# Outer products of keys and values: one head at a time in column halves, behind the chunk's value products, into the even heads' score bank

## The chip, the core and the metric

The kernel runs on one core of a Trainium2 chip. The metric is the device time of one execution in microseconds (us). TensorE, written PE in the profile, multiplies matrices: it loads a stationary operand (LDWEIGHTS, the rows PEld), streams a moving operand past it (MATMUL), and writes PSUM, eight banks of 2 KB in each of 128 partitions. VectorE (DVE) and ScalarE (ACT) read PSUM and SBUF, GpSimd (POOL) works on SBUF, and SyncE (SP) issues the DMAs. Engines wait for one another on semaphores.

## The reference, cut to what matters

Inputs are q, k, v and alpha of shape (4 batches, 8 heads, 768 steps, 48), and the weights of two feed-forward layers. All is float32.

```
for t in range(S):
    state = alpha[:, :, t, :, None] * state + np.einsum('bhd,bhe->bhde', k[:, :, t], v[:, :, t])
    y[:, :, t] = np.einsum('bhd,bhde->bhe', q[:, :, t], state)
x = y laid out as (3072 tokens, 384)
x = (sigmoid(x @ w_gate) * (x @ w_val)) @ w_out          # 384 -> 1536 -> 384
out = maximum(maximum(x @ w1, x @ w2), x @ w3) @ w_out2  # 384 -> 768 -> 384
```

## The kernel before

**Attention by chunks.** The recurrence runs in chunks of 128 steps (24 chunks; six make a batch). For a chunk, VectorE clamps alpha and scans it to running products (`decay`), and takes reciprocals (`rdec`); GpSimd multiplies q by `decay` and k by `rdec`. TensorE then does five things. `scores` multiplies k by q in each of the eight heads, even heads into bank `ps_sc`, odd heads into `ps_sc_odd`. `transposes` turns k from feature-major to token-major in PSUM, and ScalarE copies it to `khs`. `outer` multiplies `khs` by v, which is the sum over the chunk of outer products k v. `attend` adds two products into `ps_y`: q times the incoming `state` (L775), and v times the masked scores `probs` (L779). VectorE's `masked` makes `probs`, and its `new_state` adds the outer products to the state and multiplies by the decay at the chunk's end. ScalarE copies `ps_y` to the input of the next layer (`y_copy`).

**Two heads side by side.** Heads sit in pairs: one in partitions 0 to 47, one in partitions 64 to 111, with a gap of 16. `outer` takes a pair in one matmul: 112 columns of `khs` as stationary operand, 96 columns of v as moving operand. Half of what it computes (the key of one head by the value of the other) is not read. The products of L779 go one head at a time: 48 columns of v are stationary, and the two heads of a pair write partitions 0 to 47 and 64 to 111 of one bank, so each uses one half of the array's columns. The same split is in `HALVES`.

**The layers.** The first layer works on tiles of 384 tokens (three chunks), eight tiles. A tile has 12 steps f = 0 to 11. A step is 9 matmuls for the gate (`ps_gate`), 9 for the value (`ps_val`), and 9 for the output of the step before (`out1`, L815, into `ps_out`); each product is made of a high and a low part of the operands, hence w_hi, w_lo, x_hi, x_lo. Into tiles 0 to 6 the attention of the next tile's three chunks is woven: behind the gate product of steps 2, 5 and 8 come `scores` and `transposes`, behind the value product of the same steps comes `outer`, and behind the value product of steps 3, 6 and 9 comes `attend`. That is 21 chunks; the first three are done ahead of tile 0. Tile 0 is written out, tiles 1 to 6 are three turns of a loop over two tiles, tile 7 is written out. Then comes the second layer, six tiles of 512 tokens.

**What sets the order.** Each engine's program is written by hand in order, and the engines meet on counted semaphores: `y_done` (attend), `u_done` (outer), `state_done` (two for each new_state), `y_evac` (y_copy), `khs_done` (the copy of k). In the loop `transposes`, `outer` and `attend` all use the bank `ps_y`, so `attend` waits for the new_state of its own chunk. SyncE loads chunk C into the buffer of chunk C-2 as soon as the `attend` of chunk C-2 is done.

Of the kernel before, what the change touches and what calls it, by code (L numbers as in the profile page):

```python
# [32 lines left out]
B, H, S, D = 4, 8, 768, 48  # L33
# [25 lines left out]
def build(nc, att_in, alpha_flat, vT, w1, w2, consts, y, out):  # L59
    with ExitStack() as ctx:  # L60
# [76 lines left out]
        def buf(Cs):  # L137

            return 2 if Cs == 2 else Cs % 2
# [10 lines left out]
        def v_cols(b, lo, n):  # L150
            return buf_cols(b, ATT + lo, n)

        def u_bank(Cs, i):

            if isinstance(i, int) and Cs < CPT:
                return ps_out[:, 1, :]
            return ps_y.rearrange("p a t -> p (a t)")

        def arrived(eng, sems, Cs, i):

            if Cs == 2:
                eng.wait_ge(sems[2], 16)
            elif Cs < 2:
                eng.wait_ge(sems[Cs], 16)
            else:
                eng.wait_ge(sems[Cs % 2], (Cs // 2 + Cs % 2 + 3 * i) * 16)
# [38 lines left out]
        def _(sp):  # L205
            def load_chunk(Cs, i):
                b, a = buf(Cs), PAIRS * CH
                if isinstance(i, int) and Cs in (3, 4):
                    sp.wait_ge(y_done, 5 - Cs)
                elif not (isinstance(i, int) and Cs < 3):  # L210
                    sp.wait_ge(y_done, Cs + 6 * i - 1)
                sp.dma_start(buf_cols(b, 0, a), att_in[Cs + 6 * i][:, 0:a]).then_inc(alpha_loaded[b], 16)
                sp.dma_start(buf_cols(b, a, INC - a), att_in[Cs + 6 * i][:, a:INC]).then_inc(att_loaded[b], 16)

# [104 lines left out]
            for j in range(NF2):  # L319
                if j >= 2:  # L320
                    sp.wait_ge(w2_hi_done, j - 1)
                    sp.wait_ge(w2_lo_done, j - 1)
                else:
                    sp.wait_ge(y_done, CHUNKS)
                sp.dma_start(inbuf[:, (j % 2) * INC:(j % 2) * INC + W2C], w2[j]).then_inc(stage2_in[j % 2], 16)
            with sp.Fori(0, TILES2 - 1) as T:
                sp.wait_ge(o_evac, T * SUB + SUB)
# [209 lines left out]
        def _(dve):  # L537
# [38 lines left out]
            def new_state(Cs, i):  # L576

                C, cur, new = Cs + 6 * i, Cs % 2, (Cs + 1) % 2
                dve.wait_ge(u_done, C + 1)
                dve.wait_ge(end_done, C + 1)  # L580
                for n, r in enumerate(HALVES):
                    u = u_bank(Cs, i)[r, 0:PAIRS * 2 * D].rearrange("p (a e) -> p a e", a=PAIRS)[:, :, n * D:(n + 1) * D]
                    end = d_end[r, cur, :].rearrange("p (a e) -> p a e", e=1).broadcast_to([D, PAIRS, D])
                    e = slice(r.start, r.stop)
                    if Cs % (2 * CPT) == 0:
                        nc.vector.tensor_tensor(state[r, new, :, e], u, end, ALU.mult).then_inc(state_done, 1)
                        continue
                    dve.wait_ge(state_done, 2 * C)
                    nc.vector.tensor_tensor(stmp[r, :, :], u, state[r, cur, :, e], ALU.add).then_inc(stmp_done, 1)
                    later = Cs - Cs // (2 * CPT) - 1 + 5 * i  # L590
                    dve.wait_ge(stmp_done, 2 * later + n + 1)
                    nc.vector.tensor_tensor(state[r, new, :, e], stmp[r, :, :], end, ALU.mult).then_inc(state_done, 1)
# [11 lines left out]
            def layer1(Ts, i, att_next):  # L604
                T = Ts + 2 * i
                C0 = CPT * (Ts + 1)
                for f in range(NF1):
                    g = T * NF1 + f
                    c = f // 3
                    att = (C0 + c, i) if att_next and c < CPT else None  # L610
                    if att and f % 3 == 0:
                        scans(*att)
                        recips(*att, (0,))
                    elif att and f % 3 == 1:
                        recips(*att, (3,))
                    elif att:
                        masked(*att, 0)
                        masked(*att, 1)
                    dve.wait_ge(val_done, g + 1)
                    dve.wait_ge(sig_done, g + 1)  # L620
                    dve.wait_ge(h_lo_done, g)
                    nc.vector.tensor_tensor(h_sb[:, :], act_sb[:, :], ps_val[:, 0:TOK], ALU.mult).then_inc(h_done, 1)  # L622
                    if f == NF1 - 1:
                        for k in range(KT):
                            x_rest(k, (T + 1) * KT + k, *((x_raw[:, k, :],) if att_next else (mid_tile2(0, k), TOK2)))
                    h_rest(f, h_hi_done, h_lo_done, g, h_sb[:, :], TOK)
                    if att and f % 3 == 0:
                        recips(*att, (1, 2))
                    elif att and f % 3 == 2:
                        new_state(*att)  # L630

            def general():
                with dve.Fori(0, B * PAIRS) as n:
# [89 lines left out]
        def _(pe):  # L723
            mm = nc.tensor.matmul

            def transposes(Cs, i):
                C, par = Cs + 6 * i, Cs % 2
                pe.wait_ge(kh_done, 2 * C + 2)
                if not (isinstance(i, int) and Cs == 0):
                    pe.wait_ge(state_done, 2 * C)  # L730
                if not (isinstance(i, int) and Cs < CPT):
                    pe.wait_ge(y_evac, C)
                for p in range(PAIRS):
                    ins = nc.tensor.transpose(u_bank(Cs, i)[:, p * PR:(p + 1) * PR], att(buf(Cs), K)[:, p, :],  # L734
                                              ident[0:PR, 0:PR])
                ins.then_inc(tr_done, 1)

            def scores(Cs, i):

                C = Cs + 6 * i  # L740
                pe.wait_ge(qh_done, C + 1)
                if not (isinstance(i, int) and Cs == 0):
                    pe.wait_ge(mask_done, 2 * C)
                for p in range(PAIRS):
                    if p % 2 == 0:
                        pe.wait_ge(kh_done, 2 * C + p // 2 + 1)
                    for r, bank in zip(HALVES, (ps_sc, ps_sc_odd)):
                        ins = mm(bank[:, p * CH:(p + 1) * CH], att(buf(Cs), K, r)[:, p, :],  # L748
                                 att(buf(Cs), Q, r)[:, p, :], start=True, stop=True)
                ins.then_inc(sc_done, 1)  # L750

            def outer(Cs, i):

                C, par = Cs + 6 * i, Cs % 2
                pe.wait_ge(khs_done, C + 1)
                for p in range(PAIRS):
                    ins = mm(u_bank(Cs, i)[0:PR, p * 2 * D:(p + 1) * 2 * D], khs[:, p * PR:(p + 1) * PR],  # L757
                             v_cols(buf(Cs), p * 2 * D, 2 * D), start=True, stop=True)
                ins.then_inc(u_done, 1)

            def attend(Cs, i):

                C, par = Cs + 6 * i, Cs % 2
                first = Cs % (2 * CPT) == 0
                pe.wait_ge(mask_done, 2 * C + 2)
                if not (isinstance(i, int) and Cs == 0):
                    pe.wait_ge(y_evac, C)
                if isinstance(i, int) and Cs < CPT:
                    if not first:
                        pe.wait_ge(state_done, 2 * C)  # L770
                else:
                    pe.wait_ge(state_done, 2 * C + 2)
                if not first:
                    for p in range(PAIRS):
                        mm(ps_y[0:PR, p, :], state[0:PR, par, p, :], att(buf(Cs), Q)[:, p, :],  # L775
                           start=(p == 0), stop=False, skip_group_check=True)
                for p in range(PAIRS):
                    for n, r in enumerate(HALVES):
                        ins = mm(ps_y[r, p, :], v_cols(buf(Cs), (2 * p + n) * D, D), probs[:, PAIRS * n + p, :],  # L779
                                 start=(first and p == 0), stop=True, skip_group_check=True)  # L780
                ins.then_inc(y_done, 1)
# [38 lines left out]
            def layer1(Ts, i, att_next, prev):  # L820
                T = Ts + 2 * i
                C0 = CPT * (Ts + 1)
                for f in range(NF1):
# [10 lines left out]
                    if not (isinstance(i, int) and g == 0):  # L834
                        pe.wait_ge(h_done, g)
                    product(ps_val[:, 0:TOK], f, DM, W1C).then_inc(val_done, 1)
                    if att_next and f in (2, 5, 8):
                        outer(C0 + (f - 2) // 3, i)
                    if att_next and f in (3, 6, 9):
                        attend(C0 + (f - 3) // 3, i)  # L840
                    if f > 0:
                        out1(Ts, i, f - 1)
                    elif prev:
                        out1(Ts - 1, i, NF1 - 1)
# [136 lines left out]
```

## Time and profile before

| | |
|---|---|
| median of 3 runs | 897.45 us (896.21 to 897.68) |
| the profiled execution | 895.64 us |
| span of its trace | 893.8 us |
| PE busy | 863.2 us (97%) |
| PEld busy | 802.5 us (90%) |
| DVE, ACT, POOL busy | 46%, 29%, 13% |

The trace was taken from one execution, whose own time is 1.8 us below the median. A row of the costliest groups gives the source line, the engine, the output and input by name, the shape (for a matmul: rows by columns of the stationary operand, then output), the count, and the busy time. One fp32 matmul of the program shows as two MATMULs and two LDWEIGHTS in the trace, so a chunk's `outer`, four matmuls in the program, is x8 there. A matmul's duration is mostly the passage through the array: matmuls that follow each other overlap, and the distance between starts says what one costs.

### The profile page before, as it was taken

What the parts mean: (1) busy time and instruction counts of PE and PEld (TensorE: products, weight loads), DVE (VectorE), ACT (ScalarE), POOL (GpSimd) and SP (SyncE); (2) the same over time, 40 slices, a digit from 0 to 9 for tenths busy, and PEclk for the clock granted to TensorE, in tenths of its full rate; (3) what the DMA queues carried; (4) which work ended last, traced back from release to release, by engine and by line L of the source; (5) the groups of instructions that cost most, each with busy time, mean ns of one, the idle gap of its engine ahead of it and who ended that gap; (6) DMA issues with size and microseconds to landing.
All of it is one profiled execution on the core that took longest, in us unless ns stands there. A gap on an engine that the chain in (4) does not pass through costs nothing.

```text
span 893.8 us, 13520 instructions
## 1 busy us (share of the span) xinstructions
PE 863.2 (97%) x5213; PEld 802.5 (90%) x5213; DVE 414.2 (46%) x730; ACT 263.0 (29%) x502; POOL 120.5 (13%) x95
## 2 busy tenths in 40 slices
PE   4499999999999999999999999999999999999997
PEld 3489999999999999999999999998888888888886
DVE  7988566366456545545646532232323223232321
ACT  4534333232332232232233233431212212121311
POOL 4355312011011111101101101610000000000000
PEclk9799999999999999999999999999999999999999
DMA  7471021021021021021021020300000000000000
GB/s 296 157 310 45 8 89 45 8 90 45 1 98 45 1 95 45 1 97 45 1 95 45 1 78 5 137 1 1 1 35 1 35 0 35 0 35 0 13 22 35
DMA packets 15602, 46.88 MB, mean 52 GB/s; under 512 B 2112, under 2 KB 6080, under 8 KB 15552
## 3 DMA queue, kind: packets, MB, share of 16 engines
q1 hardware_dynamic: 15552, 46.15, 14.4%
q8 instruction: 39, 0.64, 0.3%
q14 instruction: 11, 0.09, 0.0%
HBM read 40.24 MB, written 4.72 MB: 50 GB/s over the span
## 4 chain that ended last, share of the span: by engine, by line
PE 92%; DVE 4%; issue 1%; DMA 1%; ACT 1%; POOL 0%; SPq 0%; ACTq 0%; DVEq 0%; POOLq 0%
PE ps_out L815 17%; PE ps_gate L790 16%; PE ps_val L790 16%; PE ps_gate L796 8%; PE ps_val L796 8%; PE ps_out L888 6%; PE ps_sc L790 5%; PE ps_sc L796 3%; PE ps_sc L748 3%; PE ps_y L779 2%; PE ps_sc_odd L888 2%; PE ps_y L775 2%; PE ps_y L757 2%; PE ps_y L734 1%; DVE rdec L560 1%
## 5 line engine op out<-in xcount | busy, mean ns | idle before, releaser
L790 PE MATMUL ps_gate<-x_hi,w_hi 128*128 128x384 f32 (+1 forms) x396 | 139.8, 353 | 2.9 <-ACT x_hi L381 2.9
L790 PE MATMUL ps_val<-x_hi,w_hi 128*128 128x384 f32 (+1 forms) x396 | 140.3, 354 | 0.9 <-DVE h_sb L622 0.9
L790 PE MATMUL ps_gate<-x_hi,w_lo 128*128 128x384 f32 (+1 forms) x396 | 139.1, 351 | 0.0
L790 PE MATMUL ps_val<-x_hi,w_lo 128*128 128x384 f32 (+1 forms) x396 | 138.4, 349 | 0.0
L622 DVE TENSOR_TENSOR h_sb<-act_sb,ps_val 128x384 f32<-128x384 f32 x96 | 52.7, 549 | 148.3 <-PE ps_val L796 148.0
L796 PE MATMUL ps_gate<-x_lo,w_hi 128*128 128x384 f32 (+1 forms) x396 | 118.1, 352 | 0.0
L796 PE MATMUL ps_val<-x_lo,w_hi 128*128 128x384 f32 (+1 forms) x396 | 117.0, 349 | 0.0
L381 ACT ACTIVATE h_hi<-h_sb 128x384 fp32r<-128x384 f32 x96 | 50.4, 525 | 159.7 <-DVE h_sb L622 159.6
L422 ACT ACTIVATE act_sb<-ps_gate 128x384 f32<-128x384 f32 x96 | 47.2, 491 | 165.2 <-PE ps_gate L796 164.9
L707 DVE TENSOR_TENSOR probs<-probs,ps_val 128x512 f32<-128x512 f32 x36 | 24.7, 687 | 137.8 <-PE ps_val L796 137.8
L601 DVE TENSOR_TENSOR h_lo<-h_sb,h_hi 128x384 fp32r<-128x384 f32 x96 | 60.5, 630 | 52.0 <-ACT h_hi L381 52.0
L560 DVE RECIPROCAL rdec<-decay 112x128 f32<-112x128 f32 x96 | 83.8, 915 | 0.0
L790 PEld LDWEIGHTS ps_gate<-x_hi,w_hi 128*128 128x128 f32 x396 | 74.7, 189 | 6.9 <-issue 2.1
L790 PEld LDWEIGHTS ps_val<-x_hi,w_hi 128*128 128x128 f32 x396 | 74.5, 188 | 5.6 <-DVE h_sb L622 1.2
L790 PEld LDWEIGHTS ps_val<-x_hi,w_lo 128*128 128x128 f32 x396 | 74.5, 188 | 4.4
L796 PEld LDWEIGHTS ps_gate<-x_lo,w_hi 128*128 128x128 f32 x396 | 73.4, 189 | 5.0
L790 PEld LDWEIGHTS ps_gate<-x_hi,w_lo 128*128 128x128 f32 x396 | 74.8, 189 | 3.2
L796 PEld LDWEIGHTS ps_val<-x_lo,w_hi 128*128 128x128 f32 x396 | 73.0, 188 | 4.2
L341 POOL TENSOR_TENSOR inbuf<-inbuf,decay 112x512 f32<-112x512 f32 x23 | 29.4, 1277 | 320.3 <-DVE decay L551 315.9
L815 PE MATMUL ps_out<-h_hi,w_hi 128*128 128x384 f32 x288 | 69.5, 349 | 0.0
L815 PE MATMUL ps_out<-h_hi,w_lo 128*128 128x384 f32 x288 | 65.8, 336 | 0.0
L815 PE MATMUL ps_out<-h_lo,w_hi 128*128 128x384 f32 x288 | 65.3, 334 | 0.0
(98 smaller groups left out, 1260.7 us busy)
## 6 DMA issues: line engine op xcount, KB each, us to landing
inbuf<-att_in SPq DMA_DIRECT2D x23, 704.0 KB, 5.6
mid<-w SPq DMA_DIRECT2D x12, 576.0 KB, 9.6
inbuf<-att_in SPq DMA_DIRECT2D x23, 256.0 KB, 2.9
mid<-alpha_flat SPq DMA_DIRECT2D x8, 576.0 KB, 6.3
inbuf<-w SPq DMA_DIRECT2D x6, 768.0 KB, 4.2
out<-inbuf SPq DMA_DIRECT2D x5, 768.0 KB, 3.5
x_raw<-y_last SPq DMA_DIRECT2D x48, 24.0 KB, 1.9
out<-inbuf SPq DMA_DIRECT2D x4, 192.0 KB, 2.1
```

Of the source, the lines that this page charges most:

```text
L341: nc.gpsimd.tensor_tensor(att(buf(Cs), Q), att(buf(Cs), Q), decay[0:PR, par], ALU.mult).then_inc(qh_done, 1)
L381: return nc.scalar.activation(o, i_, ACT.Copy)
L422: nc.scalar.activation(act_sb[:, :], ps_gate[:, 0:TOK], ACT.Sigmoid).then_inc(sig_done, 1)
L560: nc.vector.reciprocal(rdec[0:PR, Cs % 2, p, :], decay[0:PR, Cs % 2, p, :]).then_inc(rdec_done, 1)
L601: nc.vector.tensor_tensor(h_lo[:, f % 2, 0:w], h, h_hi[:, f % 2, 0:w].bitcast(F32), ALU.subtract).then_inc(lo_done, 1)
L622: nc.vector.tensor_tensor(h_sb[:, :], act_sb[:, :], ps_val[:, 0:TOK], ALU.mult).then_inc(h_done, 1)
L707: nc.vector.tensor_tensor(act2, act2, ps_val[:, :], ALU.max).then_inc(ab_done, 1)
L748: ins = mm(bank[:, p * CH:(p + 1) * CH], att(buf(Cs), K, r)[:, p, :], att(buf(Cs), Q, r)[:, p, :], start=True, stop=True)
L790: mm(bank, w_at(half, f, c + k * P, total=total), x_hi[:, k, 0:w], start=(k == 0 and half == 0), stop=False)
L796: return mm(bank, w_at(0, f, c + k * P, total=total), x_lo[:, k, 0:w], start=False, stop=(k == KT - 1))
L815: ins = mm(ps_out[:, m, 0:TOK], w_at(wh, f, 2 * DM + m * P), h[:, f % 2, 0:TOK], start=(f == 0 and n == 0), stop=(f == NF1 - 1 and n == 2))
L888: ins = mm(out_bank[s][:, 0:DM], h[:, f % 2, s * P:(s + 1) * P], w_at(wh, f, 3 * DM, DM, W2C), start=(f == 0 and n == 0), stop=(f == NF2 - ...
```

## The change

`outer` goes one head at a time: for each pair two matmuls, with 48 columns of `khs` stationary and 48 columns of v moving, one into partitions 0 to 47 and one into partitions 64 to 111. It is called behind `attend` in steps 3, 6 and 9, no longer in steps 2, 5 and 8. Its result goes to `ps_sc` in the woven chunks (`outer_bank`), and to the bank it had before in the first three. VectorE's `new_state` moves one step later, behind the reciprocals 1 and 2 of the next chunk. `attend` no longer waits for the new_state of its own chunk but for that of the chunk before; `scores` waits for the new_state of the chunk before, since it writes `ps_sc`. SyncE's load of a chunk waits on `u_done` where it waited on `y_done`.

```diff
+        def outer_bank(Cs, i):
+            if isinstance(i, int) and Cs < CPT:
+                return u_bank(Cs, i)
+            return ps_sc
...
-                    sp.wait_ge(y_done, Cs + 6 * i - 1)
+                    sp.wait_ge(u_done, Cs + 6 * i - 1)
...
+                    done = (C0 + c - 1, i) if att_next and f % 3 == 0 and c > 0 else None
...
                     if att and f % 3 == 0:
                         recips(*att, (1, 2))
-                    elif att and f % 3 == 2:
-                        new_state(*att)
+                    if done:
+                        new_state(*done)
...
             def scores(Cs, i):
+                if not (isinstance(i, int) and Cs < CPT):
+                    pe.wait_ge(state_done, 2 * C)
...
                 for p in range(PAIRS):
-                    ins = mm(u_bank(Cs, i)[0:PR, p * 2 * D:(p + 1) * 2 * D], khs[:, p * PR:(p + 1) * PR],
-                             v_cols(buf(Cs), p * 2 * D, 2 * D), start=True, stop=True)
+                    for n, r in enumerate(HALVES):
+                        ins = mm(outer_bank(Cs, i)[r, (2 * p + n) * D:(2 * p + n + 1) * D],
+                                 khs[:, p * PR + r.start:p * PR + r.stop],
+                                 v_cols(buf(Cs), (2 * p + n) * D, D), start=True, stop=True)
                 ins.then_inc(u_done, 1)
...
             def attend(Cs, i):
-                if isinstance(i, int) and Cs < CPT:
-                    if not first:
-                        pe.wait_ge(state_done, 2 * C)
-                else:
-                    pe.wait_ge(state_done, 2 * C + 2)
+                if not (isinstance(i, int) and Cs < CPT):
+                    pe.wait_ge(khs_done, C + 1)
                 if not first:
+                    pe.wait_ge(state_done, 2 * C)
...
-                    if att_next and f in (2, 5, 8):
-                        outer(C0 + (f - 2) // 3, i)
                     if att_next and f in (3, 6, 9):
                         attend(C0 + (f - 3) // 3, i)
+                        outer(C0 + (f - 3) // 3, i)
```

TensorE around the value product of step 2 before; L796 ends the value product, L757 is `outer`, L815 is `out1`, and the gate of step 3 follows.

```order
L796 MATMUL ps_val<-x_lo,w_hi 128x384 x2
L757 MATMUL ps_y<-inbuf,khs 112x96 [waits khs_done]
L757 MATMUL ps_y<-inbuf,khs 112x96 x3
L815 MATMUL ps_out<-h_hi,w_hi 128x384 [waits h_lo_done,h_hi_done]
L815 MATMUL ps_out<-h_hi,w_hi 128x384 x2
L815 MATMUL ps_out<-h_hi,w_lo 128x384 x3
L815 MATMUL ps_out<-h_lo,w_hi 128x384 x3
L790 MATMUL ps_gate<-x_hi,w_hi 128x384 [waits sig_done,w_lo_done,w_hi_done]
```

The same place in the changed kernel, where `out1` is L824.

```order
L805 MATMUL ps_val<-x_lo,w_hi 128x384 x2
L824 MATMUL ps_out<-h_hi,w_hi 128x384 [waits h_lo_done,h_hi_done]
L824 MATMUL ps_out<-h_hi,w_hi 128x384 x2
L824 MATMUL ps_out<-h_hi,w_lo 128x384 x3
L824 MATMUL ps_out<-h_lo,w_hi 128x384 x3
L799 MATMUL ps_gate<-x_hi,w_hi 128x384 [waits sig_done,w_lo_done,w_hi_done]
```

The four matmuls of `outer` are gone from here. In step 3 of the changed kernel L784 and L788 are the two parts of `attend`, L767 is `outer`.

```order
L805 MATMUL ps_val<-x_lo,w_hi 128x384 x2
L784 MATMUL ps_y<-inbuf,state 112x128 [waits khs_done,state_done,y_evac,mask_done]
L784 MATMUL ps_y<-inbuf,state 112x128 x3
L788 MATMUL ps_y<-probs,inbuf 48x128 x8
L767 MATMUL ps_sc<-inbuf,khs 48x48 [waits khs_done]
L767 MATMUL ps_sc<-inbuf,khs 48x48 x7
L824 MATMUL ps_out<-h_hi,w_hi 128x384 [waits h_lo_done,h_hi_done]
L824 MATMUL ps_out<-h_hi,w_hi 128x384 x2
```

The eight matmuls of L767 are new between `attend` and `out1`; all else of the step stands as before. VectorE from the rest `h_lo` of step 2 to the product `h_sb` of step 4 before: L589 and L592 are `new_state`, L543 and L551 clamp and scan the next chunk, L560 are its reciprocals.

```order
L601 TENSOR_TENSOR h_lo<-h_sb,h_hi 128x384
L589 TENSOR_TENSOR stmp<-ps_y,state 48x192
L592 TENSOR_TENSOR state<-stmp,d_end 48x4x48
L589 TENSOR_TENSOR stmp<-ps_y,state 48x192
L592 TENSOR_TENSOR state<-stmp,d_end 48x4x48
L543 TENSOR_SCALAR inbuf<-inbuf 112x512
L551 SCALAR_TENSOR_TENSOR decay<-inbuf,zero 112x128 x4
L560 RECIPROCAL rdec<-decay 112x128
L622 TENSOR_TENSOR h_sb<-act_sb,ps_val 128x384
L601 TENSOR_TENSOR h_lo<-h_sb,h_hi 128x384
L560 RECIPROCAL rdec<-decay 112x128 x3
L564 COPY d_end<-decay 112x4
```

The changed kernel from the `h_lo` of step 3 (L607) to the product of step 4 (L629).

```order
L607 TENSOR_TENSOR h_lo<-h_sb,h_hi 128x384
L566 RECIPROCAL rdec<-decay 112x128 x2
L595 TENSOR_TENSOR stmp<-ps_sc,state 48x192
L598 TENSOR_TENSOR state<-stmp,d_end 48x4x48
L595 TENSOR_TENSOR stmp<-ps_sc,state 48x192
L598 TENSOR_TENSOR state<-stmp,d_end 48x4x48
L566 RECIPROCAL rdec<-decay 112x128
L570 COPY d_end<-decay 112x4
L629 TENSOR_TENSOR h_sb<-act_sb,ps_val 128x384
```

The four instructions of `new_state` left the front of step 3 and stand between the third and the fourth reciprocal.

## Rows read from the trace of the kernel before

**Rows 1.** The page: engines, granted clock in 40 slices, chain by engine.
```profile
PE 863.2 (97%) x5213; PEld 802.5 (90%) x5213; DVE 414.2 (46%) x730; ACT 263.0 (29%) x502; POOL 120.5 (13%) x95
...
PEclk9799999999999999999999999999999999999999
...
PE 92%; DVE 4%; issue 1%; DMA 1%; ACT 1%; POOL 0%; SPq 0%; ACTq 0%; DVEq 0%; POOLq 0%
```

**Rows 2.** Timeline of PE, a step with `outer`: start, duration, instruction, count.
```profile
304.95 0.51 PE L796 MATMUL ps_val<-x_lo,w_hi 128*128 128x384 f32 x2
305.30 0.93 PE L757 MATMUL ps_y<-inbuf,khs 128*112 128x96 f32 x8
...
306.62 0.34 PE L815 MATMUL ps_out<-h_hi,w_lo 128*128 128x384 f32 x1
```

**Rows 3.** The same, a step without attention.
```profile
317.23 0.51 PE L796 MATMUL ps_val<-x_lo,w_hi 128*128 128x384 f32 x2
317.57 0.68 PE L815 MATMUL ps_out<-h_hi,w_hi 128*128 128x384 f32 x3
318.09 0.33 PE L815 MATMUL ps_out<-h_hi,w_lo 128*128 128x384 f32 x1
```

**Rows 4.** Source line L757: duration ns min/median/max, first and last start.
```profile
L757 PE MATMUL ps_y<-inbuf,khs x168: 244/262/262, 58.7 to 515.6; 128*112 128x96 f32 x168
```

**Rows 5.** Timeline of PE, a step with `attend`.
```profile
310.79 1.04 PE L775 MATMUL ps_y<-inbuf,state 112*112 112x128 f32 x8
311.75 1.08 PE L779 MATMUL ps_y<-probs,inbuf 128*48 128x128 f32 x16
312.77 0.79 PE L815 MATMUL ps_out<-h_hi,w_hi 128*128 128x384 f32 x3
```

**Rows 6.** The same stretch cut by narrower windows: L775 alone, L779 pair by pair.
```profile
311.55 0.27 PE L775 MATMUL ps_y<-inbuf,state 112*112 112x128 f32 x1
...
312.12 0.71 PE L779 MATMUL ps_y<-probs,inbuf 128*48 128x128 f32 x10
...
312.23 0.61 PE L779 MATMUL ps_y<-probs,inbuf 128*48 128x128 f32 x8
```

**Rows 7.** Timeline of PEld: the weight loads of L779.
```profile
311.75 0.83 PEld L779 LDWEIGHTS ps_y<-probs,inbuf 128*48 128x48 f32 x16
```

**Rows 8.** Timeline of PE, step 3 of tile 0, and the same of its second chunk.
```profile
63.83 0.51 PE L796 MATMUL ps_val<-x_lo,w_hi 128*128 128x384 f32 x2
64.59 1.10 PE L775 MATMUL ps_y<-inbuf,state 112*112 112x128 f32 x8 [0.24 <-DVE state L592]
...
82.89 0.51 PE L796 MATMUL ps_val<-x_lo,w_hi 128*128 128x384 f32 x2
83.34 1.10 PE L775 MATMUL ps_y<-inbuf,state 112*112 112x128 f32 x8
```

**Rows 9.** Timeline of DVE from step 2's rest to step 4, steady loop.
```profile
288.51 0.34 DVE L589 TENSOR_TENSOR stmp<-ps_y,state 48x192 f32<-48x192 f32 x1
...
290.06 0.43 DVE L543 TENSOR_SCALAR inbuf<-inbuf 112x512 f32<-112x512 f32 x1
...
294.38 2.57 DVE L560 RECIPROCAL rdec<-decay 112x128 f32<-112x128 f32 x3
...
299.17 0.55 DVE L622 TENSOR_TENSOR h_sb<-act_sb,ps_val 128x384 f32<-128x384 f32 x1 [2.19 <-PE ps_val L796]
```

**Rows 10.** Timeline of POOL there, and PE where the next scores begin.
```profile
297.03 0.73 POOL L345 TENSOR_TENSOR inbuf<-inbuf,rdec 112x256 f32<-112x256 f32 x1 [0.89 <-DVE rdec L560]
...
302.18 0.37 PE L748 MATMUL ps_sc<-inbuf 48*128 48x128 f32 x1
```

**Rows 11.** Timeline of PE: first gate matmul of a step 2 and of its step 3.
```profile
300.53 0.33 PE L790 MATMUL ps_gate<-x_hi,w_hi 128*128 128x384 f32 x1
...
307.67 0.33 PE L790 MATMUL ps_gate<-x_hi,w_hi 128*128 128x384 f32 x1
```

**Rows 12.** Window of the start: busy us of PE, PEld, DVE, ACT, POOL, then granted clock.
```profile
39.70:46.40 6.70, 3.33 (x10) 3.06 (x11) 6.07 (x11) 2.62 (x4) 2.62 (x1) 0.50 0.52 178
```

More of the change, by code:

```diff
@@ L323, in _ @@
                 else:
-                    sp.wait_ge(y_done, CHUNKS)
+                    sp.wait_ge(u_done, CHUNKS)
                 sp.dma_start(inbuf[:, (j % 2) * INC:(j % 2) * INC + W2C], w2[j]).then_inc(stage2_in[j % 2], 16)
@@ L581, in new_state @@
                 for n, r in enumerate(HALVES):
-                    u = u_bank(Cs, i)[r, 0:PAIRS * 2 * D].rearrange("p (a e) -> p a e", a=PAIRS)[:, :, n * D:(n + 1) * D]
+                    u = outer_bank(Cs, i)[r, 0:PAIRS * 2 * D].rearrange("p (a e) -> p a e", a=PAIRS)[:, :, n * D:(n + 1) * D]
                     end = d_end[r, cur, :].rearrange("p (a e) -> p a e", e=1).broadcast_to([D, PAIRS, D])
@@ L728, in transposes @@
                 pe.wait_ge(kh_done, 2 * C + 2)
-                if not (isinstance(i, int) and Cs == 0):
-                    pe.wait_ge(state_done, 2 * C)
                 if not (isinstance(i, int) and Cs < CPT):
                     pe.wait_ge(y_evac, C)
+                elif Cs > 0:
+                    pe.wait_ge(state_done, 2 * C)
                 for p in range(PAIRS):
@@ L767, in attend @@
                     pe.wait_ge(y_evac, C)
-                if isinstance(i, int) and Cs < CPT:
-                    if not first:
-                        pe.wait_ge(state_done, 2 * C)
-                else:
-                    pe.wait_ge(state_done, 2 * C + 2)
+                if not (isinstance(i, int) and Cs < CPT):
+                    pe.wait_ge(khs_done, C + 1)
                 if not first:
+                    pe.wait_ge(state_done, 2 * C)
                     for p in range(PAIRS):
```

## The prediction

> **What bounds the kernel now.** I read the page first: PE is busy for 97% of the span and carries 92% of the chain that ended last, at full granted clock from the third slice on; VectorE is at 46% [rows 1]. So in the woven part an instruction of TensorE costs its place in the queue, and work of other engines costs nothing unless TensorE waits for it. Next comes the timeline of PE. A step with `outer` [rows 2] is to be laid beside a step without attention [rows 3]: between the last two value matmuls and the fourth matmul of `out1` lie 306.62 - 304.95 = 1.67 us with `outer`, and 318.09 - 317.23 = 0.86 us without. One `outer` thus costs 0.81 us of TensorE. It never waits in the loop: its 168 matmuls last 244 to 262 ns each [rows 4]. The last view is the step with `attend` [rows 5, 6], since `outer` goes behind it.
>
> **What goes.** 21 woven chunks x 0.81 us = 17.0 us come off the steps 2, 5 and 8.
>
> **What is added.** In the trace each matmul counts twice, so `outer` becomes 16 MATMULs with 48 stationary and 48 moving columns, in 8 pairs of column halves. No row shows a matmul so short, so I bound the distance between pairs. The old `outer` has 112 stationary and 96 moving columns: (0.93 - 0.26) / 7 = 0.096 us from start to start [rows 2, 4]. L775 has 112 stationary and 128 moving columns: (1.04 - 0.27) / 7 = 0.110 us [rows 5, 6]. L779 has 48 stationary and 128 moving columns; its pairs are 312.23 - 312.12 = 0.11 us apart, two matmuls in that time [rows 6]. So the stream costs 0.110 / 128 = 0.86 ns a column, and where it is the shorter one, the weight load shows: 0.096 / 112 = 0.86 ns a column. The two lie beside each other, and so do the two halves. With 48 of each, the floor of a pair is 48 x 0.86 = 0.041 us, or 8 x 0.041 = 0.33 us for a chunk. The ceiling from the nearest row is the pair of L779 unshortened: 8 x 0.11 = 0.88 us. I take 0.045 us a pair, a little above the floor, because both operands of L779 and L775 scale as these rows say and the handover of some ns between equally long streams is what they can't show; 8 x 0.045 = 0.36 us a chunk, 21 x 0.36 = 7.6 us.
>
> Going from full width to halves costs 311.75 - 311.55 = 0.20 us from start to start, where matmuls of L775 otherwise stand 0.11 apart, and coming back to `out1` costs something of that sort too [rows 5, 6]. `attend` pays both now; `outer` stands between them in the same shape as L779, so it adds no third turn. In steps 2, 5 and 8 it was full width between full-width products, so it paid none either.
>
> The 16 weight loads of L779 begin at 311.75 and end at 312.58, inside the 1.08 us of its matmuls [rows 5, 7], so they hide although both halves use all 128 rows. The Trainium skill, TensorE: Matmul & The Clock Gate, section Part 3: Packing small matmuls, says that a weight load overlaps matmuls in flight only when its row group differs. By that rule L779's pairs would be 0.041 + 0.11 = 0.15 us apart; the trace shows 0.11 and disagrees. The Trainium skill, TensorEngine Tiling (Array Packing), section Instruction Overhead, speaks against the change: every matmul carries about 60 cycles, and one should not tile a dimension that is already small. Worked out from that page's figure, an estimate, 60 cycles at 2.4 GHz are 25 ns for each of 16 matmuls, 0.40 us a chunk; the sum would be 0.8 us worse. No run here shows it yet.
>
> **The wait that goes.** In tile 0 `attend` stood behind its own new_state: 64.59 - 63.83 = 0.76 us from the last two value matmuls to L775, against 0.35 us between such neighbours elsewhere (317.23 to 317.57), so 0.41 us of wait; the second chunk shows 0.45, so 0.10 us, and the third the same [rows 3, 8]. That is 0.6 us. In the loop no such wait shows. What is late next at these places is the mask, made a step earlier, so nothing.
>
> **VectorE and GpSimd.** new_state takes 290.06 - 288.51 = 1.55 us [rows 9]. It leaves the front of step 3, where clamp and scans then start that much earlier; it comes back ahead of the fourth reciprocal. The last reciprocal ends at 294.38 + 2.57 = 296.95 now and VectorE then idles 2.19 us before the product of step 4 [rows 9], more than 1.55 us, even with nothing gained in front. GpSimd's second half of k ends at 297.76, and the next scores begin at 302.18 [rows 10]: 4.4 us of cover for at most 1.55 us. new_state waits for `outer`, which ends some 0.5 us after L779, while two reciprocals of 2.57 / 3 = 0.86 us run. All this costs nothing; if the cover were gone, each us late at the scores would cost one us a chunk. SyncE's loads start 0.36 us later, and between them and the scans that read them lies at least a whole step 5 or 8, as long as step 2's 307.67 - 300.53 = 7.14 us [rows 11]: nothing. Behind the two new waits of `scores` and `attend` all of TensorE is queued, but both semaphores are set a step earlier.
>
> **The start.** The first three chunks get the same eight short matmuls between a full-width transpose and a full-width L775, which adds a turn or two of 0.1 us each and takes off about 0.4 us each; the chain there goes over VectorE and DMA, so I count zero. One thing may move: from 39.7 to 46.4 us the granted clock is 0.50, the level of 1.2 GHz, and the matmuls there keep PE busy for 3.33 us [rows 12]. If that stretch came to lie elsewhere, half of it, 1.7 us, could go or come. It goes into the range.
>
> **Sum.** 17.0 - 7.6 + 0.6 = 10.0 us less. Against the profiled execution, 895.64 - 10.0 = 885.6 us; the median shown is 1.8 us above that execution, so 897.45 - 10.0 = 887.4 us.
>
> **Rivals.**
> - *Weight loads come to light.* Load and stream are equally long now, and no row has that case; if the next load begins only when the stream before it is over, a pair takes 0.041 + 0.041 + 0.005 = 0.087 us, a chunk 0.70 us. 21 x (0.81 - 0.70) + 0.6 = 2.9 us: 894.5 us. For it: no such short pair in the trace. Against it: L757 and L779 overlap both [rows 2, 5, 7].
> - *A matmul costs by number, not by columns.* The 16 of L779 take 312.77 - 311.75 = 1.02 us [rows 5]. If 16 of `outer` take the same, because issue of instructions sets the pace, then 21 x (1.02 - 0.81) - 0.6 = 3.8 us more: 901.3 us, slower. The place is step 3 behind L779, and it decides from 0.10 us a pair upwards. For it: the instructions of `outer` double, and L779, L775 (0.110) and the scores all stand at some 0.11 us per slot. Against it: L757 stands at 0.096, and L779 issues two matmuls and two loads in 0.11 us where L775 issues one of each [rows 5, 6]. With pairs at 0.11 exactly it comes to 898.3 us.
> - *The change shortens `outer` but TensorE waits elsewhere.* VectorE late at step 4, or GpSimd late for the scores, would give back up to all of it: 897 us. The covers of 2.19 and 4.4 us speak against it [rows 9, 10].
>
> **How the numbers follow.** Forecast 0.79, with its own range 885.7 to 890; weight loads in sight 0.09; cost by number 0.07 (half of it near 898, half near 901); late elsewhere 0.05. About 0.2%, 1.8 us, is what a measurement can tell from no change. Faster takes the first two: 0.87. Same takes part of the last two, 0.07; slower 0.06. The range goes from 885.3 (the floor of 0.041 us a pair gives 886.7, less 1.4 us for clock and noise) up to 894.8, which takes in the weight loads.
>
> **What would show it.** The PE timeline: steps 2, 5 and 8 at 7.14 - 0.81 = 6.33 us from gate to gate [rows 11], and the new line x16 directly behind the value products of `attend`. The distance from the first of these 16 to the first of `out1` reads the disputed number: near 0.45 us the forecast, 0.8 us the weight loads, over 0.95 us the cost by number. No wait of PE on `state` in tile 0. VectorE's idle time before the product of step 4 should shrink but stay. The forecast is wrong if that distance is above 0.6 us, or if PE shows idle time before the scores.

## The result and the profile after

The changed kernel takes 893.41 us (median of 6 runs, 890.85 to 893.97) against 897.21 us before (median of 6, 895.60 to 898.38). The ratio is 0.995, with a 95% interval of 0.9938 to 0.9963. It is faster, by 3.8 us where 10.0 were forecast. The profiled execution took 890.85 us, span 889.1; against the profiled execution of before that is 4.8 us of span. It is the fastest of its six, and the other five took 893.1 to 894.0 us, so the two traces differ by 1 us more than the medians do.

The page after, its answers to [rows 1]:

```profile
PE 855.4 (96%) x5405; PEld 797.8 (90%) x5405; DVE 413.7 (47%) x730; ACT 263.2 (30%) x502; POOL 120.8 (14%) x95
...
PEclk9789999999999999999999999999999999999999
...
PE 94%; DVE 2%; issue 1%; ACT 1%; DMA 1%; POOL 0%; SPq 0%; ACTq 0%; DVEq 0%; POOLq 0%
```

TensorE is busy for 7.8 us less, and the span shrank by 4.8 us only, so some of the gain came back as idle time. The timeline of PE in the woven part, first a step 2 (it answers [rows 2]), then a step 3 (it answers [rows 5]):

```profile
302.86 0.51 PE L805 MATMUL ps_val<-x_lo,w_hi 128*128 128x384 f32 x2
303.21 0.68 PE L824 MATMUL ps_out<-h_hi,w_hi 128*128 128x384 f32 x3
...
307.89 1.04 PE L784 MATMUL ps_y<-inbuf,state 112*112 112x128 f32 x8
308.86 1.08 PE L788 MATMUL ps_y<-probs,inbuf 128*48 128x128 f32 x16
309.77 0.53 PE L767 MATMUL ps_sc<-inbuf,khs 128*48 128x48 f32 x16
310.22 0.79 PE L824 MATMUL ps_out<-h_hi,w_hi 128*128 128x384 f32 x3
```

`outer` is gone from step 2, which lasts 6.33 us from gate to gate instead of 7.14. In step 3 the 16 matmuls of L767 begin 0.11 us behind the last pair of L788 and stand (0.53 - 0.21) / 7 = 0.046 us apart by pairs, where one of them lasts 0.21 us. From the first of them to the first of `out1` are 310.22 - 309.77 = 0.45 us. The step lasts 7.13 us instead of 6.79, so `outer` costs 0.34 us there.

What gave the rest back stands where TensorE's loop over tiles turns, which happens twice. This is the timeline of PE at the first turn, before:

```profile
253.55 0.69 PE L815 MATMUL ps_out<-h_lo,w_hi 128*128 128x384 f32 x3
254.72 0.44 PE L790 MATMUL ps_gate<-x_hi,w_hi 128*128 128x384 f32 x1 [0.48 <-ACT x_hi L381]
```

The `x_hi` that the view names had long been done; this is its row in ScalarE's timeline, which ends at 253.32, 1.4 us earlier:

```profile
252.79 0.53 ACT L381 ACTIVATE x_hi<-x_raw 128x384 fp32r<-128x384 f32 x1 [1.15 <-PE ps_val L796]
```

And the same place after:

```profile
250.01 0.68 PE L824 MATMUL ps_out<-h_lo,w_hi 128*128 128x384 f32 x3
253.56 0.44 PE L799 MATMUL ps_gate<-x_hi,w_hi 128*128 128x384 f32 x1 [2.87 <-issue]
```

"issue" says that the engine waited for nothing that the profile shows as a semaphore. From the last matmul of `out1` to the gate's first is 0.82 us before and 3.21 us after, where two neighbours stand 0.17 apart. The second turn shows 0.93 and 2.91 us. What is over 0.17 is called idle time below: 0.65 and 0.76 us before, 3.04 and 2.74 us after.

The whole difference, by starts of steps in the two traces:

| | us |
|---|---|
| 21 steps 2, 5, 8: 0.81 less each, with `outer` gone | -17.0 |
| 18 steps of the loop 3, 6, 9: 0.34 more each | +6.1 |
| the 3 of tile 0: 7.24, 6.93, 6.93 now 7.13 each (0.34 more, a wait of 0.73 in all gone) | +0.3 |
| two turns of the loop: idle 0.65 and 0.76, now 3.04 and 2.74 | +4.4 |
| start, up to the first matmul of the gate in step 2 of tile 0: at 53.92, now at 55.31 | +1.4 |
| sum | -4.8 |

### The profile page after: what moved, and what is told of

Its sections match the earlier page's. It is cut to its first block, busy times and chain, and to the rows that moved or that the text cites. A ratio compares the mean times of both kernels' runs of the same rounds, so it can differ in the third digit from the quotient of the medians.

```text
span 889.1 us, 13943 instructions
## 1 busy us (share of the span) xinstructions
PE 855.4 (96%) x5405; PEld 797.8 (90%) x5405; DVE 413.7 (47%) x730; ACT 263.2 (30%) x502; POOL 120.8 (14%) x95
## 4 chain that ended last, share of the span: by engine, by line
PE 94%; DVE 2%; issue 1%; ACT 1%; DMA 1%; POOL 0%; SPq 0%; ACTq 0%; DVEq 0%; POOLq 0%
PE ps_gate L799 17%; PE ps_out L824 17%; PE ps_val L799 17%; PE ps_gate L805 8%; PE ps_val L805 8%; PE ps_out L896 6%; PE ps_sc L799 6%; PE ps_sc L805 3%; PE ps_sc L757 3%; PE ps_y L788 3%; PE ps_sc_odd L896 2%; PE ps_y L784 2%; PE ps_y L741 1%; PE ps_sc L767 1%; DVE rdec L566 1%
## 5 line engine op out<-in xcount | busy, mean ns | idle before, releaser
L629 DVE TENSOR_TENSOR h_sb<-act_sb,ps_val 128x384 f32<-128x384 f32 x96 | 52.7, 549 | 139.9 <-PE ps_val L805 139.8
L566 DVE RECIPROCAL rdec<-decay 112x128 f32<-112x128 f32 x96 | 85.7, 923 | 0.5
L607 DVE TENSOR_TENSOR h_lo<-h_sb,h_hi 128x384 fp32r<-128x384 f32 x96 | 61.2, 637 | 52.0 <-ACT h_hi L387 52.0
L824 PE MATMUL ps_out<-h_hi,w_hi 128*128 128x384 f32 x288 | 67.7, 342 | 0.0
L824 PE MATMUL ps_out<-h_hi,w_lo 128*128 128x384 f32 x288 | 65.4, 334 | 0.0
L824 PE MATMUL ps_out<-h_lo,w_hi 128*128 128x384 f32 x288 | 65.3, 334 | 0.0
```

Of the source, the lines that this page charges most:

```text
L566: nc.vector.reciprocal(rdec[0:PR, Cs % 2, p, :], decay[0:PR, Cs % 2, p, :]).then_inc(rdec_done, 1)
L607: nc.vector.tensor_tensor(h_lo[:, f % 2, 0:w], h, h_hi[:, f % 2, 0:w].bitcast(F32), ALU.subtract).then_inc(lo_done, 1)
L824: ins = mm(ps_out[:, m, 0:TOK], w_at(wh, f, 2 * DM + m * P), h[:, f % 2, 0:TOK], start=(f == 0 and n == 0), stop=(f == NF1 - 1 and n == 2))
```

## The experiments

### What happens at the turn

At the turn TensorE's sequencer executes the branch back and then needs code from the loop's start, which a DMA of 16 KB brings (queue q8, kind "instruction"). Two views of DMA show it. Before, from 251.0 to 252.6 us:

```profile
DMA packets 1, 0.02 MB, mean 10 GB/s; under 512 B 0, under 2 KB 0, under 8 KB 0
...
q8 instruction: 1, 0.02, 3.4%
```

After, from 247.5 to 250.8 us:

```profile
DMA packets 322, 1.06 MB, mean 320 GB/s; under 512 B 30, under 2 KB 30, under 8 KB 322
...
q1 hardware_dynamic: 322, 1.06, 93.4%
```

Before, the code fetch runs on idle DMA engines, 0.97 us behind the branch. After, 1.06 MB of chunk loads run first, and the fetch starts 3.36 us behind the branch. What decides is who comes first, SyncE's loads or TensorE's branch. The DMA queue's own timeline (SPq), before:

```profile
251.67 0.34 SPq L212 DMA_DIRECT2D inbuf<-att_in  x1
```

And after:

```profile
246.67 0.34 SPq L218 DMA_DIRECT2D inbuf<-att_in  x1
```

The branch is executed at 251.07 before and at 247.53 after. The loads went from 0.60 us behind it to 0.85 us ahead of it. `outer` behind `attend` accounts for 0.34 us of this: SyncE's chain starts from `attend`, and TensorE's branch now comes 0.34 us later after it. The remaining 1.1 us are SyncE's own: from the test ahead of its wait for the moved rows of y to its branch it took 2.62 us before and 1.51 us after. Before, one of TensorE's ordinary 16 KB code fetches started at 248.25, when the last small moves of y were under way. In the changed kernel, with 192 more matmuls and weight loads in the code ahead of the end of the loop (12 chunks of 16), none starts there.

Two theories went on record. A: the fetch of the loop's code queues behind the chunk loads. B: the longer code lies otherwise within the pieces of 16 KB, and that alone makes the turn slow.

### Loads held until TensorE has turned

```diff
+                    if Ts == 1:
+                        sp.wait_ge(pe_turned, i + 1)
                     for c in range(CPT):
                         load_chunk(CPT * (Ts + 1) + c, i)
...
             with pe.Fori(0, (TILES - 2) // 2) as i:
+                pe.sem_inc(pe_turned, 1)
```

> The changed kernel, with SyncE's first chunk load of each loop turn held until TensorE has passed the loop's turn. In the changed kernel's trace the two turns cost 3.0 and 2.7 us of TensorE, before 0.7 each; SyncE's loads are issued 0.85 us ahead of TensorE's branch there, and 0.60 us behind it before. Theory A (the fetch of the loop's code queues behind the chunk loads): each turn falls back to 0.7 us or so, 4.4 us less in all, about 889.0 us, if VectorE bears the later loads. Theory B (the doubled matmuls moved the loop's start and end within the pieces of 16 KB in which code is fetched, and that alone makes the turn slow): the turns stay near 2.9 us, 893.4 us.

Measured 887.94 us, ratio to before 0.9899 (0.9884 to 0.9914). The code of `outer` and the woven order are the changed kernel's. Timeline of PE at the first turn:

```profile
248.97 0.69 PE L827 MATMUL ps_out<-h_lo,w_hi 128*128 128x384 f32 x3
250.21 0.44 PE L802 MATMUL ps_gate<-x_hi,w_hi 128*128 128x384 f32 x1 [0.56 <-ACT x_hi L390]
```

Both turns are back at 0.72 us of idle time, and 5.5 us of run time are gone by the medians. Theory A holds, and theory B, which had 893.4 us for this code, does not. The later loads have a price: VectorE waits for the first chunk, and TensorE for VectorE, once a turn in the second step of the tile, which is 0.57 and 0.43 us longer. One row of VectorE's timeline and one of TensorE's:

```profile
253.49 0.43 DVE L552 TENSOR_SCALAR inbuf<-inbuf 112x512 f32<-112x512 f32 x1 [2.31 <-DMA inbuf<-att_in]
...
256.88 0.44 PE L802 MATMUL ps_val<-x_hi,w_hi 128*128 128x384 f32 x1 [0.16 <-DVE h_sb L632]
```

### No turn at all, after and before

```diff
-            with pe.Fori(0, (TILES - 2) // 2) as i:
+            for i in range((TILES - 2) // 2):
```

> The changed kernel with TensorE's loop over tiles written out, so that it has no turn. Both theories of the turn: 3.0 + 2.7 us of idle time go, 893.4 - 5.8 = 887.6 us, which is the forecast of the prediction. If the steps of the loop were slower in other executions than in the profiled one, it stays above 890 us.

> The kernel before with the same loop written out. Its turns cost 0.65 and 0.75 us in the trace: 897.2 - 1.4 = 895.8 us. With the changed kernel so written at 887.6 us the change would be worth 8.2 us where no loop turns; if this one comes to 891 us or less, the turn of the loop is not where the change loses.

Measured 885.77 us for the changed kernel (ratio to before 0.9871, 0.9856 to 0.9886) and 895.51 us for the one before (0.9979, 0.9970 to 0.9988). Where no loop turns, the change is worth 895.51 - 885.77 = 9.7 us. The forecast was 10.0. In both traces every step at which the turn was is 4.68 us. By the medians the loop cost the changed kernel 893.41 - 885.77 = 7.6 us, 1.9 more than the 5.8 us of idle time in its trace, and by that much the 887.6 expected was too high; the kernel before lost 1.9 us, with 1.4 us of idle time. Part of the difference may be what the second profile of the changed kernel shows below; the slower executions have no trace.

### Halves alone, in the old place

The edit is that of `outer` in the diff of the change, with `u_bank`, in the kernel before. Nothing is moved.

> The kernel before with only the matmuls of outer changed to one head at a time in column halves, in their old place and bank. The trace of the changed kernel has outer behind attend at 0.34 us. Here two changes of tile shape come in, some 0.1 to 0.2 us each: 0.55 to 0.7 us against 0.81, so 21 x 0.1 to 0.26 = 2 to 5.5 us less in the woven steps, and the wait in tile 0 stays. Its code is as long as the changed kernel's, but TensorE reaches the turn no later after attend than before. Theory A: SyncE's loads are not early by outer's 0.34 us, the turns cost at most 1 to 2 us. Theory B: the turns cost 2.9 us each as in the changed kernel.

Measured 896.51 us, ratio 0.9995 (0.9986 to 1.0004): no difference. Timeline of PE around `outer`:

```profile
305.29 0.51 PE L798 MATMUL ps_val<-x_lo,w_hi 128*128 128x384 f32 x2
305.73 0.56 PE L758 MATMUL ps_y<-inbuf,khs 128*48 128x48 f32 x16
306.22 0.79 PE L817 MATMUL ps_out<-h_hi,w_hi 128*128 128x384 f32 x3
306.85 0.33 PE L817 MATMUL ps_out<-h_hi,w_lo 128*128 128x384 f32 x1
```

From the last two value matmuls to the fourth of `out1` is 306.85 - 305.29 = 1.56 us, against 0.86 without `outer` [rows 3]. The short matmuls cost 0.70 us here, the upper end of what was expected, and 0.34 us behind `attend`. The same 16 matmuls are 0.36 us dearer a chunk where they stand between full-width products. A change of the array's shape, for them and back, is the likely reason and was not tested by itself: 0.09 of the 0.36 us shows ahead of the first of them, which starts 0.44 us behind the last two value matmuls where the full-width `outer` started 0.35 us behind them [rows 2]. The rest is in the matmuls themselves and in coming back to `out1`, which `attend` pays anyway in the other place. The turns cost 1.06 and 1.76 us of idle time, with loads 0.5 to 0.6 us ahead of the branch. Theory B, which had 2.9 us here for the same length of code, misses again. But the loads did get ahead though nothing was moved: SyncE took 1.51 us to its branch here too. The turns took 1.4 us of the 2.3 us that the halves gave.

### The move alone, full width

The edit is the whole change with the old four matmuls in `outer`:

```diff
-                    for n, r in enumerate(HALVES):
-                        ins = mm(outer_bank(Cs, i)[r, (2 * p + n) * D:(2 * p + n + 1) * D],
-                                 khs[:, p * PR + r.start:p * PR + r.stop],
-                                 v_cols(buf(Cs), (2 * p + n) * D, D), start=True, stop=True)
+                    ins = mm(outer_bank(Cs, i)[0:PR, p * 2 * D:(p + 1) * 2 * D], khs[:, p * PR:(p + 1) * PR],
+                             v_cols(buf(Cs), p * 2 * D, 2 * D), start=True, stop=True)
```

> The changed kernel with its moves (outer behind attend, into the score bank, new_state a step later) but with the old full-width matmuls. A step 2 should fall to 6.33 us as in the changed kernel, a step 3 should gain the old price of outer, 0.8 us, so the woven steps are as before but for the 0.6 us of waiting that go in tile 0. Its code is as long as the kernel's before. Theory A (SyncE's chunk loads against the fetch of TensorE's loop code): TensorE reaches the turn 0.8 us later after the last attend than before, the loads get ahead, each turn costs 1 to 3 us against 0.7: 897 to 901 us. Theory B (position of the code): turns of 0.7 us, 896.6 us.

Measured 898.11 us, ratio 1.0006 (0.9997 to 1.0015): no difference. Timeline of PE in a step 3:

```profile
312.62 1.08 PE L786 MATMUL ps_y<-probs,inbuf 128*48 128x128 f32 x16
313.63 1.03 PE L766 MATMUL ps_sc<-inbuf,khs 128*112 128x96 f32 x8
314.44 0.42 PE L822 MATMUL ps_out<-h_hi,w_hi 128*128 128x384 f32 x1
```

Step 3 lasts 7.57 us, 0.78 more than before, and step 2 is down by 0.81. The move by itself brings 0.03 us a chunk. With the experiment before it, that divides the 0.47 us: the halves alone bring 0.81 - 0.70 = 0.11, the place alone 0.03, and the other 0.33 come only with both. The turns cost 1.32 and 1.75 us, with code as long as before and loads 0.45 and 0.27 us ahead of the branch, as theory A had it; theory B had 0.7 us each.

### The changed kernel once more

> The changed kernel once more, unaltered, for a second profile. The first profiled execution took 890.85 us, the others of that kernel 893.1 to 894.0. If the turns of the loop vary, they cost more here than 3.0 and 2.7 us, up to 2.5 us more in all; if the start varies (the granted clock was 0.50 from 33.3 to 50.3 us in the first profile, 0.50 from 40.0 to 46.8 us in the run whose loads wait for the turn, with the same code up to there), the first step of tile 0 is between 6.8 and 8.1 us.

Measured 892.05 us, ratio 0.9948 (0.9935 to 0.9961), the same result as the first time. Its turns cost 1.58 and 2.72 us of idle time. So the turns do vary, but not the way expected: they cost less here than in the first profile, and the profiled execution (891.08 us) is again the fastest of its six. Behind the second the windows show one more cost (columns: PE, PEld, DVE, ACT, POOL busy us, then granted clock, DMA share and GB/s):

```profile
391.00:394.30 3.30, 2.93 (x9) 2.94 (x10) 2.18 (x5) 0.00 (x0) 1.28 (x1) 0.50 0.10 37
394.40:398.00 3.60, 3.60 (x22) 3.60 (x21) 1.28 (x3) 1.24 (x3) 0.00 (x0) 1.00 0.02 5
```

TensorE had idled for 2.7 us, and the granted clock was 0.50, its level of 1.2 GHz, from 390.9 to 394.3 us: that step lasts 6.12 us where it lasts 4.8 in the other profile. There the idle times of 3.04 and 2.74 us were followed by full clock. So a slow turn can cost 1.3 us more than its idle time, and does not always.

All turns seen, by the records of TensorE's branch, of the first load and of the first code fetch behind the branch (us; load and fetch relative to the branch; first turn, second turn):

| kernel | first load | fetch starts | idle of TensorE |
|---|---|---|---|
| loads held | +3.72, +3.71 | +0.94, +0.99 | 0.72, 0.72 |
| before | +0.60, +0.49 | +0.97, +1.00 | 0.65, 0.76 |
| full width moved | -0.45, -0.27 | +1.63, +2.09 | 1.32, 1.75 |
| halves in place | -0.51, -0.59 | +1.33, +1.63 | 1.06, 1.76 |
| after, second profile | -0.86, -0.93 | +1.88, +3.10 | 1.58, 2.72 |
| after | -0.85, -0.93 | +3.36, +3.12 | 3.04, 2.74 |

At the four turns where the loads came behind the branch, the fetch started 0.94 to 1.00 us after it. At the eight where they came ahead, it started 1.33 to 3.36 us after it. The order within the second kind is not strict, so how long the fetch waits also hangs on something else, which stays open.

### A busier start

The loop written out, and transposes of the identity into the idle gate bank, whose results are not read:

```diff
+            def keep_busy(n):
+                for _ in range(n):
+                    nc.tensor.transpose(ps_gate[:, 0:P], ident, ident)
...
                 outer(c, 0)
+                if c == 1:
+                    keep_busy(6)
                 attend(c, 0)
+            keep_busy(8)
```

> The changed kernel with TensorE's loop written out, and 14 transposes of the identity into the idle gate bank added where TensorE waits at the start: 6 ahead of the second attend, 8 behind the third. Their results are not read. If the granted clock of 0.50 after 40 us follows from TensorE's idle time before it, the first product runs at full clock: 1.0 to 2.5 us less than the 885.8 us of the loop written out, about 884 us. If the clock falls all the same, or the transposes come in the way, 885.8 us or up to 2 us more.

Measured 884.85 us (884.76 to 884.90), ratio 0.9862 (0.9847 to 0.9876). The granted clock still fell to 0.50, from 41.4 to 48.3 us, so the reason given for this edit is not borne out; the time lies between the two that were expected. The gate of step 2 starts at 55.16 us against 55.81 without the transposes. It is the lowest median of the study, 12.7 us below the median before of its own comparison (897.57), but its lead of 0.9 us on the written-out loop lies within the two intervals.

## Why the prediction was wrong

**The price of `outer` and its new one were right.** 0.81 us came off 21 steps. The disputed distance between pairs was 0.046 us against 0.045, and from the first of the 16 to `out1` it was the 0.45 us named for the forecast. The chunk cost 0.34 us against 0.36, for the last pair hands over to `out1` in 0.45 - 7 x 0.046 = 0.13 us, where the last pair of L779 took 1.02 - 7 x 0.11 = 0.25 before. The rule of the Trainium skill on weight loads of one row group (TensorE: Matmul & The Clock Gate, Part 3: Packing small matmuls), which [rows 7] already went against, fails here too: pairs of 48 stationary columns stand 0.046 us apart, far below the 0.087 of a load and a stream one behind the other. The 60 cycles per matmul, estimated at 0.40 us a chunk from the Trainium skill, TensorEngine Tiling (Array Packing), section Instruction Overhead, did not bind, though not by much: 8 pairs x 0.046 = 0.37 us, and 0.34 us net. The sentence of the forecast that `outer` adds no third change of shape was right and worth more than it said: the experiment with the halves in place puts the two changes, if it is they that cost, at 0.36 us a chunk, where the text had 0.20 instead of 0.11 us for one direction, so 0.09.

**The wait in tile 0 went.** 0.73 us by the steps, 0.6 forecast; L784 follows the value product of step 3 without idle time.

**VectorE and GpSimd had the cover.** In the timeline of DVE after, a chunk with reciprocals, new_state stands between them and 1.37 us of idle time are left of the 2.19:

```profile
291.57 1.76 DVE L566 RECIPROCAL rdec<-decay 112x128 f32<-112x128 f32 x2
293.24 0.29 DVE L595 TENSOR_TENSOR stmp<-ps_sc,state 48x192 f32<-48x192 f32 x1
...
294.73 0.95 DVE L566 RECIPROCAL rdec<-decay 112x128 f32<-112x128 f32 x1
295.60 0.11 DVE L570 COPY d_end<-decay 112x4 f32<-112x4 f32 x1
297.07 0.56 DVE L629 TENSOR_TENSOR h_sb<-act_sb,ps_val 128x384 f32<-128x384 f32 x1 [1.37 <-PE ps_val L805]
```

**The step that failed** is "SyncE's loads start 0.36 us later [...]: nothing". The sum put nothing for the turns of the loop, and they took 4.4 us more of idle time than before (0.65 and 0.76 us, now 3.04 and 2.74). The sentence "It never waits in the loop" rests on the durations of `outer`'s matmuls [rows 4], which say nothing of the gap at the turn. I asked whether the loads come in time for their readers. I did not ask what else shares the DMA engines when they run. The trace before had the answer half open: an idle 0.65 us of TensorE at 254 us with a code fetch beside it, in a loop otherwise without such gaps. The loads came 0.60 us behind the branch there, and the cover was never counted. It was not the loads that moved later but the branch, by the 0.34 us of `outer`, while SyncE came 1.1 us earlier. The rival "TensorE waits elsewhere" named VectorE and GpSimd, with 0.05; the wait was for code. That the range, up to 894.8, holds the time is luck: it reached so far for weight loads in sight, which did not come. The likeliest number was 6.0 us off, and the gain was 3.8 us of 10.0. (The chances have a slip too: the first two add up to 0.88, not 0.87.)

**The start.** The gate of step 2 starts 1.4 us later in the first profile after, whose granted clock was 0.50 from 33.3 to 50.3 us, where it was 0.50 from 39.6 to 46.5 before. The prediction had 1.7 us either way for this. It is not a cost of the change as far as the runs show: the gate of step 2 of tile 0 started at 55.31, 55.66, 54.26 and 55.81 us in four executions with the same code up to there, and at 53.92 and 55.26 us in two of the old code. It goes with the clock: in the three traces of the study whose half-clock stretch ends by 47.5 us that gate starts at 53.9 to 54.7 us, and in the six where it ends between 48.3 and 50.6 us, at 55.2 to 55.9 us.

**What stays open.** Why SyncE took 1.1 us less to its branch was read from the traces (no code fetch beside the last moves of y), and no experiment was made for it. It fits all profiles: 2.4 to 2.6 us in the two kernels that had such a fetch there, 1.5 us in the others. The nearest thing to a test is the kernel before with TensorE's loop written out: SyncE's code is the old one, the fetches fall elsewhere (at 235.1 and 259.1 us), and SyncE takes 1.51 us. So theory B had a grain of truth. The longer code does not make the turn slow by itself, but by where its fetches fall it lets the loads come earlier. Open are also what sets the fetch's delay between 1.33 and 3.36 us behind loads, and what the executions slower than the profiled one lost.

## What to carry to other kernels

A small matmul that computes only what is read can cost less than half of a wide one, but only beside others of its tile shape: here 0.34 us behind the value products of `attend` and 0.70 us between full-width products, against 0.81 us for the wide form (0.78 behind `attend`). When an edit moves the long engine against the DMA issuer, look at each turn of a loop for the code fetch, and see which bulk transfers stand ahead of it; a loop of few turns can be written out (7.6 us here), or the loads held until the branch is past (5.5 us). A gap of under 1 us that the profile puts down to "issue", or to a producer long done, is worth a look before it is taken for noise.

## What the runs showed of the hardware that was not expected

- A branch back over a long loop on TensorE took 3.3 to 3.5 us where the DMA engines were free, with a 16 KB code fetch starting 0.94 to 1.00 us behind it, and up to 5.8 us behind chunk loads. TensorE's queued work hides all but 0.7 us of the first.
- Two matmuls in column halves with 48 stationary and 48 moving fp32 columns each took 0.046 us a pair. At the 0.86 ns a column of the wider matmuls 48 columns are 0.041 us.
- Sixteen such matmuls between full-width ones cost 0.36 us more than behind matmuls of their own shape (0.70 against 0.34 us).
- One idle time of 2.7 us was followed by 3.4 us at half clock; others of 2.7 and 3.0 us were not.
- SyncE's wait for its last small moves took 2.4 to 2.6 us with a 16 KB code fetch of TensorE beside them, 1.5 us without.
